# Routing chain reordered, filler matmuls on TensorE, the slot loop turned round, and own tiles for the last slot

## The chip, the cores and the metric

The kernel runs on one core of one Trainium2 chip. The metric is device microseconds (us) of one execution, as the median of several. Engines are named as in the profile: PE is TensorE (PEld its weight loads), DVE VectorE, ACT ScalarE, POOL GpSimd, SP SyncE.

## The reference

Three layers follow each other. A delta-rule attention layer gives `x` (3072 tokens of 384), a dense feed-forward layer gives `x1`, and a mixture of eight experts with one expert for each token gives the output:

```
for t in range(S):                                   # attention: 4 x 8 heads, 768 steps, state 48x48
    y[:, :, t] = q[:, :, t] @ state
    state = state + beta * outer(k_n, v - state @ k_n)
h = np.maximum(x @ w_in, 0.0);  x1 = h * h @ w_out   # 384 -> 2048 -> 384
logits = x1 @ w_gate;  e = argmax(logits)            # 8 experts
out[token] = softmax(logits)[e] * (relu(x1[token] @ w1[e]) @ w2[e])    # 384 -> 1024 -> 384
```

The gate's weight is positive, so the kernel multiplies the rows of `x1` by it before the expert layer.

## The kernel before, in words

Everything is written out by hand: each engine has its own program, and semaphores alone order the engines. Matmuls in fp32r are done in three passes (high times high, high times low, low times high), so each operand has a high part (ACT copies it with rounding) and a low part (DVE or POOL subtract).

The first part, `front`, runs over six chunks of 512 tokens. While PE works through the 16 blocks of the dense layer for chunk t (`up`, `down`, 18 matmuls a block), the delta rule of chunk t+1 is woven in. After each chunk's sum the tokens are routed: `sums` (ACT) copies the three result banks to `x1T`, `gate_logits` (PE) makes the logits, `choose` and `gates` (DVE) pick an expert and the gate, `ranks` (PE) counts tokens before each one, `places` (DVE) makes the token's place within its expert, `turn` (PE) and `turned` (ACT) turn the rows back and scale them, and SP stores them in HBM (`store_x1`). For chunks 0 to 4 this lies beside the next chunk's blocks. For chunk 5 nothing is left to lie beside: PE, DVE and ACT wait for each other in the order logits, `choose`, `ranks`, `places`, `slots`, `lists`.

`slots` (DVE) lays each expert's tokens into slots of 128 rows, 31 in all: it counts the slots that each expert needs (`need`, `end`, `begin`), gives each token its slot (`slot`) and builds one-hot matrices `parts` (24 columns of 128 tokens, 32 slots) in three groups of 8 columns. `mark_spots` (DVE) builds the other one-hot factor, `here` (a token's row within its slot, times its number); chunks 0 to 2 are marked in the last chunk's first blocks, chunks 3 and 4 behind its last block, chunk 5 between the groups of `parts`. `lists` (PE) multiplies the two, 24 matmuls into one bank, and DVE turns the sum into `ids`, the token numbers of each slot. `x_slot`, `rows` and the expert layer follow from it: POOL gathers the rows of slot 0, 1, 2, ... by `ids` (`gather`), and for each slot PE turns the rows (`turn_x`), ACT and DVE split them (`x_hi`, `x_lo`), PE runs `up` (18 matmuls of 512 columns), ACT the relu, PE turns the result (`turn_h`, 8 transposes), ACT and DVE split it (`h_hi`, `h_lo`), PE runs `down` (24 matmuls of 384 columns), ACT copies the result to `rows` and POOL scatters it. PE's loop body for slot s is `up(s)`, `turn_x(s+1)`, `down(s-1)`, `turn_h(s)`, so the small steps of one slot lie beside the matmuls of another.

The weights of experts 0 and 1 are loaded during the last chunks and split by `expert_hi` (ACT, one piece of 768 columns behind a block) and `expert_lo` (POOL, as soon as the piece is there). SP issues the raw weights of expert 2 as soon as those splits are done and the rows of chunk 5 are stored.

## Time and profile before

| | us |
|---|---|
| median of 3 runs | 988.73 (988.29 to 989.4) |
| the profiled execution, its own time | 986.88 |
| its span in the trace | 985.2 |
| PE busy | 895.5 of the span |
| DVE busy | 468.7 |
| ACT busy | 426.7 |
| POOL busy | 195.0 |

PE's busy time says that some matmul was in flight, not that it ran at its full speed: matmuls overlap, and their ends are modelled. What a stage costs is read from the distance between starts. The profiled execution is 1.85 us below the median, and its span is 1.68 us below its own time.

### The profile page before, as it was taken

How to read it: one execution, taken by the hardware profiler on the slowest of the kernel's cores; microseconds unless marked ns; L12 is line 12 of the kernel's file. 1: busy time of each engine (PE TensorE's matmuls, PEld its weight loads, DVE VectorE, ACT ScalarE, POOL GpSimd, SP SyncE). 2: the span in 40 equal slices, each digit the busy share in tenths (PEclk: the TensorE clock that was granted, in tenths of full speed). 3: DMA queues.
4: the chain of work that ended last, by engine and by line, in shares of the span. 5: the costliest groups of instructions: out<-in, count | busy, mean ns of one | idle time of the engine just before them, and what ended most of it. 6: DMA issues, size and time to landing. Idle time of an engine off the chain costs nothing.

```text
span 985.2 us, 25990 instructions
## 1 busy us (share of the span) xinstructions
PE 895.5 (91%) x10379; PEld 767.9 (78%) x10380; DVE 468.7 (48%) x953; ACT 426.7 (43%) x745; POOL 195.0 (20%) x146
## 2 busy tenths in 40 slices
PE   3161999999999999999999999986999999999997
PEld 3161788788877888888888888865989898899987
DVE  6989679746744675467422144152232323232221
ACT  4051746753566347534633555641333333333332
POOL 3000000000000000000000013335676623376311
PEclk8575899999999999999999999986999999999999
DMA  7005558933864377437633796607567733361100
GB/s 315 1 16 212 195 178 301 387 133 131 280 225 132 109 277 266 130 126 235 200 128 100 249 358 222 226 33 231 145 238 282 254 137 136 128 257 73 63 23 6
DMA packets 36893, 175.85 MB, mean 179 GB/s; under 512 B 4574, under 2 KB 7812, under 8 KB 30914
## 3 DMA queue, kind: packets, MB, share of 16 engines
q1 hardware_dynamic: 30242, 144.83, 41.3%
q0 software_dynamic: 6560, 29.70, 8.6%
q8 instruction: 71, 1.16, 0.5%
q14 instruction: 20, 0.16, 0.0%
HBM read 147.76 MB, written 28.12 MB: 179 GB/s over the span
## 4 chain that ended last, share of the span: by engine, by line
PE 85%; DVE 9%; issue 2%; ACT 2%; DMA 1%; POOL 0%; DVEq 0%; POOLq 0%; ACTq 0%
PE HP L1104 7%; PE ACC L1117 7%; PE HP L1105 6%; PE HP L1106 6%; PE ACC L1118 6%; PE ACC L1119 6%; PE HP L1442 5%; PE HP L1443 4%; PE HP L1444 4%; PE ACC L1467 4%; PE ACC L1468 4%; PE ACC L1469 4%; PE P L1008 3%; PE P L1453 3%; DVE prod L676 2%
## 5 line engine op out<-in xcount | busy, mean ns | idle before, releaser
L356 POOL TENSOR_TENSOR we_l<-raw_e,we_h 128x768 fp32r<-128x768 f32 x16 | 31.0, 1941 | 615.1 <-ACT we_h L482 615.1
L725 DVE TENSOR_TENSOR h_l<-h,h_h 128x512 fp32r<-128x512 f32 x96 | 66.3, 690 | 175.3 <-ACT h_h L456 175.2
L448 ACT ACTIVATE relu<-HP 128x512 f32<-128x512 f32 x96 | 57.4, 598 | 201.1 <-PE HP L1106 200.7
L1104 PE MATMUL HP<-x_h,ring 128*128 128x512 f32 x288 | 119.1, 414 | 0.6 <-DVE x_l L718 0.6
L1117 PE MATMUL ACC<-h_h,ring 128*128 128x512 f32 x288 | 117.2, 407 | 0.6 <-DVE h_l L725 0.6
L1105 PE MATMUL HP<-x_h,ring 128*128 128x512 f32 x288 | 113.4, 394 | 0.4 <-issue 0.4
L1106 PE MATMUL HP<-x_l,ring 128*128 128x512 f32 x288 | 113.4, 394 | 0.0
L1118 PE MATMUL ACC<-h_h,ring 128*128 128x512 f32 x288 | 113.1, 393 | 0.0
L1119 PE MATMUL ACC<-h_l,ring 128*128 128x512 f32 x288 | 112.9, 392 | 0.0
L1392 DVE TENSOR_TENSOR hT_l<-P,hT_h 128x512 fp32r<-128x512 f32 x62 | 40.0, 686 | 101.7 <-ACT hT_h L1346 101.7
L1297 POOL TENSOR_TENSOR we_l<-raw_e,we_h 128x1536 fp32r<-128x1536 f32 (+2 forms) x24 | 83.8, 3514 | 21.9 <-DMA we_h<-in_w 21.4
L1467 PE MATMUL ACC<-we_h,hT_h 128*128 x248 | 86.0, 347 | 1.3 <-DVE hT_l L1392 1.3
L1468 PE MATMUL ACC<-we_l,hT_h 128*128 x248 | 83.6, 337 | 0.0
L1469 PE MATMUL ACC<-we_h,hT_l 128*128 x248 | 83.4, 336 | 0.0
L1442 PE MATMUL HP<-we_h,xT_h 128*128 x186 | 77.3, 416 | 2.4 <-DVE xT_l L1385 2.3
L1339 ACT ACTIVATE h_slot<-HP 128x512 f32<-128x512 f32 x62 | 37.2, 600 | 95.9 <-PE HP L1444 95.1
L1443 PE MATMUL HP<-we_l,xT_h 128*128 x186 | 74.5, 400 | 0.0
L1444 PE MATMUL HP<-we_h,xT_l 128*128 x186 | 74.4, 400 | 0.0
L1385 DVE TENSOR_TENSOR xT_l<-ACC,xT_h 128x384 fp32r<-128x384 f32 x31 | 17.3, 558 | 119.5 <-ACT xT_h L1333 119.5
L1104 PEld LDWEIGHTS HP<-x_h,ring 128*128 128x128 f32 x288 | 54.5, 189 | 13.9 <-issue 2.6
L1117 PEld LDWEIGHTS ACC<-h_h,ring 128*128 128x128 f32 x288 | 54.4, 189 | 13.3 <-DVE h_l L725 1.0
L1350 ACT ACTIVATE rows<-ACC 128x384 f32 (+1 forms) x31 | 15.2, 491 | 113.9 <-PE ACC L1469 113.9
(195 smaller groups left out, 1719.7 us busy)
## 6 DMA issues: line engine op xcount, KB each, us to landing
ring<-w_scratch SPq DMA_DIRECT2D x80, 768.0 KB, 4.8
raw_e<-in_w SPq DMA_DIRECT2D x16, 1536.0 KB, 7.0
w_scratch<-ring SPq DMA_DIRECT2D x16, 768.0 KB, 5.3
we_h<-in_w POOLq DMA_DIRECT2D x6, 1536.0 KB, 9.2
kT<-in_kT SPq DMA_DIRECT2D x6, 1024.0 KB, 8.9
kk<-in_k SPq DMA_DIRECT2D x6, 1024.0 KB, 8.2
qT<-in_qT SPq DMA_DIRECT2D x6, 1024.0 KB, 9.6
we_h<-in_w POOLq DMA_DIRECT2D x6, 1024.0 KB, 6.1
```

The costliest lines, as they stand in the source:

```text
L1104: pe.matmul(HP[n % 2][:, :], win_h[:, cols], x_h[:, k, :], start=k == 0, stop=False)
L1105: pe.matmul(HP[n % 2][:, :], win_l[:, cols], x_h[:, k, :], start=False, stop=False)
L1106: last = pe.matmul(HP[n % 2][:, :], win_h[:, cols], x_l[:, k, :], start=False, stop=k == KD - 1)
L1117: pe.matmul(ACC[m][:, :], wout_h[:, cols], h_h[n % 2][:, :], start=f == 0, stop=False)
L1118: pe.matmul(ACC[m][:, :], wout_l[:, cols], h_h[n % 2][:, :], start=False, stop=False)
L1119: last = pe.matmul(ACC[m][:, :], wout_h[:, cols], h_l[n % 2][:, :], start=False, stop=f == NF1 - 1)
L1442: pe.matmul(HP[n][:, :], xT_h[:, lhs], wh[:, cols], start=k == 0, stop=False)
L1443: pe.matmul(HP[n][:, :], xT_h[:, lhs], wl[:, cols], start=False, stop=False)
L1444: last = pe.matmul(HP[n][:, :], xT_l[:, lhs], wh[:, cols], start=False, stop=k == KD - 1)
L1467: pe.matmul(YP[:, 0:DM], hT_h[:, lhs], wh[:, cols], start=f == 0, stop=False)
L1468: pe.matmul(YP[:, 0:DM], hT_h[:, lhs], wl[:, cols], start=False, stop=False)
L1469: last = pe.matmul(YP[:, 0:DM], hT_l[:, lhs], wh[:, cols], start=False, stop=f == NF2 - 1)
```

## The change

On DVE, `places` is split: `count` adds a chunk's counts to `filled`, and for the last chunk it comes alone before `slots`. `slots` then makes `begin`, and a new `give_slots` works on ranges of columns: 0 to 7, 8 to 19, and 20 to 23 (the last chunk). Only ahead of the third range stand `places(5)` and `mark_spots(5)`. `mark_spots` uses four tensor_scalar instructions of 128 elements instead of two tensor_tensor instructions of 512. Chunks 3 and 4 are marked behind the last two blocks. On ACT the last four pieces of `expert_hi` go behind blocks 13 and 14, two each.

On PE, the last chunk's logits are ordered by k-block instead of by batch, so that they may start when the first of three copies is there. `stay_awake` is new: matmuls of a high part with itself into bank ACC[2], whose result nobody reads. There are 3 of 512 columns behind the logits, 10 of 512 and 25 of 64 ahead of `lists`, and 74 of 64 behind it. `LIST` moves to bank ACC[0]. `lists` waits for the groups of 8, 12 and 4 columns.

SP's first load for expert 2 also waits for the first gathered slot.

In the expert layer PE's loop starts with `turn_h`, and `turn_h` of the last slot stands in the middle of the `down` of the slot before it. The last slot's hidden rows and its result have tiles and a bank of their own, so nothing waits for the other slot's buffers.

```diff
+HTL0, Y0 = 2, 1
+SHORT = (25, 74)
...
-    LIST = AUX[:, 0:NS]
+    LIST = ACC[0][:, 0:NS]
...
-            elif t == NCH and f >= 9:
+            elif t == NCH and 9 <= f < 13:
                 expert_hi(f - 1)
-        expert_hi(15)
+            elif t == NCH and f in (13, 14):
+                for i in range(2 * f - 14, 2 * f - 12):
+                    expert_hi(i)
...
+        def count(t):
+            dve.wait_ge(ranked, t + 1)
+            then(dve.tensor_tensor(filled[(t + 1) % 2][:, :], filled[t % 2][:, :], ADD, ALU.add))
+
         def places(t):
 
-            dve.wait_ge(ranked, t + 1)
+            if t < NCH - 1:
+                count(t)
...
-            then(dve.tensor_tensor(filled[(t + 1) % 2][:, :], filled[t % 2][:, :], ADD, ALU.add))
...
-            mine = here[t // KD][:, n:n + B, :]
-            then(dve.tensor_tensor(mine, spots[:, :].unsqueeze(1).broadcast_to([128, B, 128]),
-                                   spot[:, B * t:B * (t + 1)].unsqueeze(2).broadcast_to([128, B, 128]), ALU.is_equal))
-            dve.tensor_tensor(mine, mine.bitcast(F32), token[:, B * t:B * (t + 1)].unsqueeze(2).broadcast_to([128, B, 128]),
-                              ALU.mult).then_inc(here_done, 1)
+            for c in range(B * t, B * (t + 1)):
+                last = dve.tensor_scalar(here[t // KD][:, n + c - B * t, :], spots[:, :], spot[:, c:c + 1],
+                                         token[:, c:c + 1], ALU.is_equal, ALU.mult)
+            last.then_inc(here_done, 1)
+
+        def give_slots(begin, lo, hi):
+
+            n, cols = hi - lo, slice(lo, hi)
+            mine = relu[1][:, 0:n * NE].rearrange("p (c e) -> p c e", e=NE)
+            then(dve.tensor_tensor(mine, picked[:, cols, :].bitcast(F32), begin.unsqueeze(1).broadcast_to([128, n, NE]),
+                                   ALU.mult))
+            then(dve.tensor_reduce(slot[:, cols], mine, AX.X, ALU.add))
+            then(dve.tensor_tensor(slot[:, cols], slot[:, cols], line[:, cols], ALU.add))
+            dve.tensor_tensor(parts[:, cols, :], slot[:, cols].unsqueeze(2).broadcast_to([128, n, NS]),
+                              slot_no[:, :].unsqueeze(1).broadcast_to([128, n, NS]), ALU.is_equal).then_inc(parts_done, 1)
...
             dve.wait_ge(up_done, NF1 * NCH)
-            for n in range(0, NCOL, NLIST):
...
+            give_slots(begin, 0, NLIST)
+            give_slots(begin, NLIST, NCOL - B)
+            places(NCH - 1)
+            mark_spots(NCH - 1)
+            give_slots(begin, NCOL - B, NCOL)
...
+            if t == NCH and f >= 14:
+                dve.wait_ge(x1_out, 16 * NCH)
+                mark_spots(f - 11)
...
-        dve.wait_ge(x1_out, 16 * NCH)
-        for t in range(KD, NCH - 1):
-            mark_spots(t)
         choose(NCH - 1)
         gates(NCH - 1)
-        places(NCH - 1)
+        count(NCH - 1)
         slots()
...
+        def stay_awake(n, columns=TILE):
+
+            for _ in range(n):
+                pe.matmul(ACC[2][:, 0:columns], h_h[1][:, 0:128], h_h[1][:, 0:columns], start=True, stop=True)
...
-                if c % NLIST == 0:
-                    pe.wait_ge(parts_done, c // NLIST + 1)
-                    pe.wait_ge(here_done, NCH if c == NCOL - NLIST else NCH - 1)
+                if c in (0, NLIST, NCOL - B):
+                    pe.wait_ge(here_done, NCH - 1 if c < NCOL - B else NCH)
+                    pe.wait_ge(parts_done, 1 if c == 0 else 2 if c == NLIST else 3)
...
-        for b in range(B):
-            gate_logits(NCH - 1, b)
+        pe.wait_ge(placed, NCH - 1)
+        for m in range(KD):
+            pe.wait_ge(x1T_done, KD * (NCH - 1) + m + 1)
+            for b in range(B):
+                last = pe.matmul(AUX[:, DM + NE * b:DM + NE * (b + 1)], x1T[:, m, C * b:C * (b + 1)], wg[:, m, :],
+                                 start=m == 0 and b == 0, stop=m == KD - 1 and b == B - 1)
+        last.then_inc(lg_done, B)
+        stay_awake(3)
...
+        stay_awake(10)
+        stay_awake(SHORT[0], 64)
         lists()
...
+        stay_awake(SHORT[1], 64)
...
                 sp.wait_ge(lo_done, NPIECE * e + 2 * n + 2)
+                if e == 2:
+                    sp.wait_ge(first_rows[0], 16)
...
+        def last_h_hi():
+            for n in range(2):
+                act.wait_ge(ht_done, 2 * (NSLOT - 1) + n + 1)
+                act.activation(last_hh[n][:, :], TP[n][:, :], ACT.Copy).then_inc(hth_done, 1)
...
+        last_h_hi()
         result(NSLOT - 2)
-        h_hi(NSLOT - 1)
-        result(NSLOT - 1)
+        result(NSLOT - 1, last_YP)
...
+                if f == 4 and between is not None:
+                    turn_h(between)
...
-        turn_h(0)
-        with pe.Fori(1, NSLOT - 1) as s:
-            up(s, slot_expert(s))
-            turn_x(s + 1)
-            down(s - 1, slot_expert(s - 1))
+        with pe.Fori(0, NSLOT - 2) as s:
             turn_h(s)
+            up(s + 1, slot_expert(s + 1))
+            turn_x(s + 2)
+            down(s, slot_expert(s))
+        turn_h(NSLOT - 2)
         up(NSLOT - 1, slot_expert(NSLOT - 1))
-        down(NSLOT - 2, slot_expert(NSLOT - 2))
-        turn_h(NSLOT - 1)
-        down(NSLOT - 1, slot_expert(NSLOT - 1))
+        down(NSLOT - 2, slot_expert(NSLOT - 2), between=NSLOT - 1)
+        down(NSLOT - 1, slot_expert(NSLOT - 1), bank=last_YP, last_tiles=last_h)
```

PE's program from the last chunk's logits to the first slot, before (AUX, P, HP and ACC are PSUM banks; L1130 the logits, L1152 `turn`, L1140 to L1144 `ranks`, L1163 `lists`, L1423 `turn_x(0)`):

```order
L1130 MATMUL AUX<-wg,x1T 128x8 x12
L1152 MATMUL P<-ident,x1T 128x128 x6
L1140 MATMUL AUX<-picked,upper 128x32
...
L1144 MATMUL AUX<-picked,ones_sq 128x8 x4
L1152 MATMUL HP<-ident,x1T 128x128 x6
L1163 MATMUL AUX<-parts,here_x 128x32 x24
L1412 UNCONDITIONAL_BRANCH
L1423 MATMUL ACC<-ident,rows 128x128 x3
```

The same place in the changed kernel:

```order
L1262 MATMUL AUX<-wg,x1T 128x8 x12
L1169 MATMUL ACC<-h_h 128x512 x3
L1163 MATMUL P<-ident,x1T 128x128 x6
L1151 MATMUL AUX<-picked,upper 128x32
...
L1155 MATMUL AUX<-picked,ones_sq 128x8 x4
L1163 MATMUL HP<-ident,x1T 128x128 x6
L1169 MATMUL ACC<-h_h 128x512 x10
L1169 MATMUL ACC<-h_h 128x64 x25
L1179 MATMUL ACC<-parts,here_x 128x32 x24
L1169 MATMUL ACC<-h_h 128x64 x74
L1451 UNCONDITIONAL_BRANCH
L1462 MATMUL ACC<-ident,rows 128x128 x3
```

Three blocks of fillers now stand in PE's queue, one behind the logits, one ahead of `lists` and one between `lists` and the first slot.

DVE's program from the ranks of the last chunk to `ids`, before, is in this order (L770 to L778 `places`, L802 to L812 the slots, L818 `parts`, L786 and L788 `mark_spots`):

```order
L770 TENSOR_TENSOR rank<-AUX,filled 128x32
L772 TENSOR_TENSOR filled<-filled,AUX 128x8
...
L802 TENSOR_TENSOR relu<-filled,steps 128x192
...
L809 TENSOR_TENSOR relu<-picked,relu 128x192
L811 TENSOR_REDUCE slot<-relu 128x24
L812 TENSOR_TENSOR slot<-slot,line 128x24
L818 TENSOR_TENSOR parts<-slot,slot_no 128x256 x2
L786 TENSOR_TENSOR here_x<-spots,spot 128x512
L788 TENSOR_TENSOR here_x<-here_x,token 128x512
L818 TENSOR_TENSOR parts<-slot,slot_no 128x256
```

In the changed kernel it is this (L802 to L806 `give_slots`, L779 to L786 `places`, L794 `mark_spots`):

```order
L770 TENSOR_TENSOR filled<-filled,AUX 128x8
L819 TENSOR_TENSOR relu<-filled,steps 128x192
...
L802 TENSOR_TENSOR relu<-picked,relu 128x64
...
L806 TENSOR_TENSOR parts<-slot,slot_no 128x256
...
L806 TENSOR_TENSOR parts<-slot,slot_no 128x384
L779 TENSOR_TENSOR rank<-AUX,filled 128x32
...
L786 SCALAR_TENSOR_TENSOR spot<-line,place 128x4
L794 TENSOR_SCALAR here_x<-spots,spot,token 128x128 x4
...
L806 TENSOR_TENSOR parts<-slot,slot_no 128x128
```

The places of the last chunk moved from ahead of the slots to behind the first two groups of `parts`, and the last group shrank from 256 to 128 elements.

## Rows read from the trace of the kernel before

**Rows 1.** The page, clock of PE granted in 40 slices, tenths.

```profile
PEclk8575899999999999999999999986999999999999
```

**Rows 2.** Timeline of PE, last chunk to slot 1: start, us, engine, line.

```profile
650.62 0.50 PE L1117 MATMUL ACC<-h_h,ring 128*128 128x512 f32 x1 [0.56 <-DVE h_l L725]
...
653.64 2.85 PE L1130 MATMUL AUX<-wg,x1T 128*128 128x8 f32 x24 [0.69 <-ACT x1T L462]
...
657.89 0.40 PE L1140 MATMUL AUX<-picked,upper 128*128 128x32 f32 x1 [0.26 <-DVE picked L753]
...
659.62 1.54 PE L1152 MATMUL HP<-ident,x1T 128*128 128x128 f32 x6
664.49 5.30 PE L1163 MATMUL AUX<-parts,here_x 128*128 128x32 f32 x24 [3.33 <-DVE parts L818]
676.38 0.88 PE L1423 MATMUL ACC<-ident,rows 128*128 128x128 f32 x3 [6.58 <-DMA rows<-x_scratch,ids]
678.81 0.79 PE L1442 MATMUL HP<-we_h,xT_h 128*128 x1 [1.55 <-DVE xT_l L1385]
...
685.43 0.49 PE L1423 MATMUL ACC<-ident,x_slot 128*128 128x128 f32 x3
...
687.68 0.50 PE L1442 MATMUL HP<-we_h,xT_h 128*128 x1 [0.75 <-DVE xT_l L1385]
```

**Rows 3.** Windows, PE alone: length, PE busy (x), PEclk, DMA share, GB/s.

```profile
656.00:657.00 1.00, 1.00 (x10) 0.81 0.00 0
...
683.50:684.00 0.50, 0.50 (x2) 0.57 0.79 194
```

**Rows 4.** Timeline of DVE, ranks of the last chunk to `ids`.

```profile
659.79 0.19 DVE L770 TENSOR_TENSOR rank<-AUX,filled 128x32 f32<-128x32 f32 x1 [1.25 <-PE AUX L1144]
...
661.32 0.35 DVE L802 TENSOR_TENSOR relu<-filled,steps 128x192 f32<-128x192 f32 x1
...
663.01 0.36 DVE L809 TENSOR_TENSOR relu<-picked,relu 128x192 f32<-128x192 f32 x1
...
664.01 0.76 DVE L818 TENSOR_TENSOR parts<-slot,slot_no 128x256 fp32r<-128x256 f32 x2
...
666.35 0.40 DVE L821 TENSOR_TENSOR h<-slot_no,relu 1x248 f32<-1x248 f32 x1
...
667.61 0.16 DVE L826 CAST control<-relu 1x8 int32<-1x8 f32 x1
669.93 0.19 DVE L828 TENSOR_SCALAR ids<-AUX 128x31 int32<-128x31 f32 x1 [2.16 <-PE AUX L1163]
```

**Rows 5.** Timeline of POOL: the first gather.

```profile
671.05 1.23 POOL L1281 DMA_INDIRECT rows<-x_scratch,ids  x1 [15.96 <-DVE ids L828]
```

**Rows 6.** The 31 gathers by their source line, from issue to landing.

```profile
DMA to landing us min/median/max: 3.0/3.2/5.2
```

**Rows 7.** Timeline of SP: the raw weights of expert 2.

```profile
665.52 0.82 SPq L1276 DMA_DIRECT2D raw_e<-in_w  x2
```

**Rows 8.** Timeline of PE, ranks of an earlier chunk, full clock.

```profile
343.23 0.59 PE L1144 MATMUL AUX<-picked,ones_sq 128*128 128x8 f32 x4
```

**Rows 9.** Timeline of POOL in the last chunk's block 14: `expert_lo`.

```profile
646.57 1.85 POOL L356 TENSOR_TENSOR we_l<-raw_e,we_h 128x768 fp32r<-128x768 f32 x1 [2.23 <-ACT we_h L482]
```

**Rows 10.** Chain that ended last, one turn of the slot loop: start, us, what.

```profile
706.24 0.87 PE P L1453 x8
707.11 0.23 PE HP L1442
...
711.31 0.33 PE ACC L1423 x3
715.82 0.87 PE P L1453 x8
```

**Rows 11.** DMA queues between 700 and 950 us: the instruction queues.

```profile
q14 instruction: 3, 0.02, 0.0%
```

**Rows 12.** Timeline of PE, the last slot's down matmuls.

```profile
976.91 0.44 PE L1467 MATMUL ACC<-we_h,hT_h 128*128 x1 [1.28 <-DVE hT_l L1392]
```

More of the change, by code:

```diff
@@ L808, in slots @@
             then(dve.tensor_tensor(begin, end, need, ALU.subtract))
-            then(dve.tensor_tensor(mine, picked[:, :, :].bitcast(F32), begin.unsqueeze(1).broadcast_to([128, NCOL, NE]),
-                                   ALU.mult))
-            then(dve.tensor_reduce(slot[:, :], mine, AX.X, ALU.add))
-            then(dve.tensor_tensor(slot[:, :], slot[:, :], line[:, :], ALU.add))
             dve.wait_ge(up_done, NF1 * NCH)
-            for n in range(0, NCOL, NLIST):
-                cols = slice(n, n + NLIST)
-                if n == NCOL - NLIST:
-                    mark_spots(NCH - 1)
-                dve.tensor_tensor(parts[:, cols, :], slot[:, cols].unsqueeze(2).broadcast_to([128, NLIST, NS]),
-                                  slot_no[:, :].unsqueeze(1).broadcast_to([128, NLIST, NS]),
-                                  ALU.is_equal).then_inc(parts_done, 1)
+            give_slots(begin, 0, NLIST)
[3 more added lines that the diff above has]
+            give_slots(begin, NCOL - B, NCOL)
             then(dve.tensor_tensor(all_past, slot_no[0:1, 0:NSLOT].unsqueeze(2).broadcast_to([1, NSLOT, NE]),
@@ L1249, in _, with expert_layer @@
             turn(NCH - 1, b, turn_bank[b])
+        stay_awake(10)
+        stay_awake(SHORT[0], 64)
         lists()
-def expert_layer(nc, ctx, block, banks, routed, tiles, experts, w1, w2, x1_scratch, ident, ids, control, out):
+        stay_awake(SHORT[1], 64)
+def expert_layer(nc, ctx, block, banks, routed, tiles, last_h, experts, w1, w2, x1_scratch, ident, ids, control, out):
     def sem(name):
@@ L1393, in h_lo, with last_h_lo @@
                                   ALU.subtract).then_inc(htl_done, 1)
+        def last_h_lo():
+            for n in range(2):
+                dve.wait_ge(hth_done, 2 * (NSLOT - 1) + n + 1)
+                dve.tensor_tensor(last_hl[n][:, :], TP[n][:, :], last_hh[n][:, :].bitcast(F32),
+                                  ALU.subtract).then_inc(htl_done, 1)
         fetch(1)
@@ L1450, in turn_h @@
                 after(pe, h_done, 2 * s + n + 1)
-                after(pe, htl_done, 2 * s - 1 + n)
+                after(pe, htl_done, 2 * s - 1 + n + HTL0)
                 for f in range(4):
@@ L1455, in turn_h, with down @@
                 last.then_inc(ht_done, 1)
-        def down(s, e):
+        def down(s, e, between=None, bank=YP, last_tiles=None):
             wh, wl = (w[:, :, :].rearrange("p b n -> p (b n)") for w in (we_h, we_l))
-            after(pe, y_done, s)
+            if last_tiles is None:
+                after(pe, y_done, s + Y0)
             at = (e & 1) * WE
             for f in range(NF2):
+                if f == 4 and between is not None:
+                    turn_h(between)
                 if f % 4 == 0:
                     pe.wait_ge(lo_done, NPIECE * e + (NPIECE + 3 + f // 4))
-                    after(pe, htl_done, 2 * s + f // 4 + 1)
-                lhs = slice(128 * f, 128 * (f + 1))
+                    after(pe, htl_done, 2 * s + f // 4 + 1 + HTL0)
+                if last_tiles is None:
+                    h_hi, h_lo = (h[:, 128 * f:128 * (f + 1)] for h in (hT_h, hT_l))
+                else:
+                    h_hi, h_lo = (h[f // 4][:, 128 * (f % 4):128 * (f % 4 + 1)] for h in last_tiles)
                 cols = bass.ds(at + (W1 + DM * f), DM)
-                pe.matmul(YP[:, 0:DM], hT_h[:, lhs], wh[:, cols], start=f == 0, stop=False)
-                pe.matmul(YP[:, 0:DM], hT_h[:, lhs], wl[:, cols], start=False, stop=False)
-                last = pe.matmul(YP[:, 0:DM], hT_l[:, lhs], wh[:, cols], start=False, stop=f == NF2 - 1)
+                pe.matmul(bank[:, 0:DM], h_hi, wh[:, cols], start=f == 0, stop=False)
+                pe.matmul(bank[:, 0:DM], h_hi, wl[:, cols], start=False, stop=False)
+                last = pe.matmul(bank[:, 0:DM], h_lo, wh[:, cols], start=False, stop=f == NF2 - 1)
             last.then_inc(slots_done, 1)
         pe.sem_inc(slots_done, 1)
+        pe.sem_inc(htl_done, HTL0)
+        pe.sem_inc(y_done, Y0)
         pe.wait_ge(routed, 2)
@@ L1511, in build @@
                  sb("hT_l", [128, F2], F32R))
+        last_h = [[sb(f"last_h{c}{n}", [128, 512], F32R) for n in range(2)] for c in ("h", "l")]
         def bank(name):
@@ L1524, in build @@
               xT_scratch, x1_scratch, ident, ids, control)
-        expert_layer(nc, ctx, block, banks, routed, tiles, experts, w1, w2, x1_scratch, ident, ids, control, out)
+        expert_layer(nc, ctx, block, banks, routed, tiles, last_h, experts, w1, w2, x1_scratch, ident, ids, control, out)
 def kernel(**inputs):
```

14 lines of the change are left out of this document (7 added, 7 removed).

## The prediction

> **What bounds the kernel now.** I read the page first. The granted clock stands at 9 or more in every slice behind the start but for three around 700 us [rows 1]: one place, between the dense layer and the expert layer, where PE is neither busy nor fast. Then the timeline of PE there [rows 2]. Between the last `down` block, which begins at 650.62, and `up(1)` at 687.68 lie only the logits, the ranks, 24 small matmuls of `lists`, one `turn_x` and `up(0)`; the rest is waiting, 3.33 us for `parts`, 6.58 us for the first gather. The windows add the clock [rows 3]: it falls within the window from 656 to 657, though PE was then busy with 24 passes of 8 columns, and is back at full in the window from 683.5. So the second half of the logits' wake, ranks, turns, `lists` and 5 us of `up(0)` run at 1.2 GHz. Behind that, the slot loop: the chain of one turn is 0.87 for `turn_h`, 4.20 for `up`, 0.33 for `turn_x`, 4.18 for `down` (each from its row's start to the next), and these fill the whole period of 9.58, 715.82 less 706.24 [rows 10]. Last, the final slot waits 1.28 us for its split [rows 12]. What can be gained is thus in the passage and at the end, hardly in the loop.
>
> **The logits and the block before them.** Ordered by k-block, the logits need one copy of `x1T` instead of three, so the wait of 0.69 ahead of them goes [rows 2]: they end at 655.8 instead of 656.49. Against this stands a price. ACT's second cast behind block 14 makes POOL run two subtractions of 1.85 from 646.57, until 650.3 [rows 9], and DVE, which now marks chunk 3 in that time, does the `h_l` that PE waits for until 650.62 [rows 2]. It was free of POOL before. Bounds: nothing, if they don't disturb each other, and 1.0, if `h_l` has to wait for POOL. I take 0.4, nearer to the first since the overlap is under half a microsecond. Logits end at 656.2.
>
> **Ranks.** From the logits' end to the first rank pass DVE chooses, 1.40 (656.49 to 657.89), unchanged: 657.6. The three wide fillers and six transposes (0.7 and 0.66 at full clock) fit before that. Ranks to DVE took 1.90 at half clock (657.89 to 659.79 [rows 2, 4]). At full clock a pass of these costs 0.113: four in 0.59, of which the last takes 0.25, in [rows 8]; eight are 0.9, with the way to DVE 1.0. DVE starts at 658.6 instead of 659.79.
>
> **DVE's chain.** Before, it runs from 659.79 to 667.77 and then waits for `lists` until 669.93 [rows 4]. Now: count 0.20; slots needed to `begin` 1.69 (661.32 to 663.01); first group 1.06 (three small steps of 0.2 to 0.26, `parts` 0.34 to the next start); second group 1.25, since it is half as wide again; the rest of `places` 1.4 (661.32 less 659.79, less count, plus one wait); four marks of 128 elements; third group 0.84; control words 1.47 (666.35 to 667.77 and the step to `ids`). The mark in this form has no row. A 192-wide instruction costs 0.36, a narrow one 0.16 [rows 4], so four lie between 0.6 and 1.5; I take 1.0. The sum is 8.9, so `ids` at 667.5 instead of 669.93, 2.4 earlier. `lists` does not hold it back: its third group may start at 666.0.
>
> **The gather.** It starts 1.12 behind `ids` (669.93 to 671.05 [rows 4, 5]), now at 668.6. Its landing took 5.2, the longest of 31, with a median of 3.2 [rows 6]; beside it ran 3 MB of raw weights issued at 665.52 [rows 7], which now wait for it. I take 3.2, between 3.0 and 5.2. Rows of slot 0 are there at 671.8, against 676.3. The raw weights start some 6 us later; their user, the split for expert 2, comes after POOL's 31 gathers of 1.3 each, so past 709, and this costs nothing; behind SP's new wait stand only the loads for experts 2 to 7.
>
> **The fillers.** These are what PE must do before `turn_x(0)`, whether or not the rows are there, for they stand ahead of it in a queue that keeps its order. From the ranks at 657.6: eight passes 0.9, six transposes 0.66, ten of 512 columns at 0.233 (the step of `up` [rows 10]) 2.33, 25 of 64 columns, `lists`, 74 of 64 columns. The price of a 64-column one decides. Passes of 8 columns cost 0.113 [rows 8], of 32 columns at half clock 0.214 (5.30 less the last, by 23 [rows 2]), so twice as much as at full: the cost does not follow the columns but the weight load, and 64 columns stay under it. Bounds: 0.06 if something of the load goes away for weights that repeat, 0.113 otherwise. I take 0.113. Then 25 end at 664.3, 20 of `lists` at 666.6, four more at 667.05, 74 (8.36 us) at **675.4**. That is 3.6 later than the rows land, so the fillers take the place of the gather as the last to end, and the shorter chain to the slots is worth only what is left, 676.38 less 675.4: **1.0**.
>
> **Slot 0 and the end.** With the clock held, `turn_x(0)` to `up(0)` (2.43) loses 0.3, since three transposes took 0.88 where 0.33 is the step at full clock, hidden in part by the copies. `up(0)` took 6.62 (678.81 to 685.43 [rows 2]) and takes 4.3, **2.3** less. From there to `up(1)` nothing changes. At the end `turn_h(30)` in the middle of `down(29)` puts 12 matmuls, 2.1 us, over ACT's and DVE's split (0.6 and 0.7 for each half); the 1.28 goes, less 0.1 for one more change between transposes and matmuls: **1.2**.
>
> **The loop.** The order of the work is the same around the cycle; only the branch moves. It can save or cost no more than the chain leaves open, under 0.02 of 9.58, so 0.6 in 29 turns; I take 0. The instruction queue of PE moved nothing between 700 and 950: of the instruction queues only q14 appears there, with three packets [rows 11], so no code is fetched again in 26 turns.
>
> The Trainium skill, page Runtime: NRT & Kernel Launch, section Instruction fetch mechanics, says that a taken branch to code outside the pages held forces a fetch and a stall. By it a loop body over two blocks might pay each turn; the trace's period leaves no room for it, and the sum stays.
>
> Sum: 1.0 + 0.3 + 2.3 + 1.2 = 4.8. The profiled execution goes from 986.88 to 982.1 (its span from 985.2 to 980.4); it stands 1.85 below the median of the runs, so 983.9 against 988.73.
>
> **The rivals.**
> *The gather ends last, not the fillers.* If a 64-column filler costs under 0.072 (5.3 us for 74, from 666.5 to 671.8), 3.6 more are gained: 980.3. For it speaks only that the same weights are loaded again each time; against it the 0.113 at every small width.
> *The fillers run at half clock.* Before the fall PE was busy with passes of 8 columns, and 5.3 us of 32-column passes of `lists` did not bring the clock back [rows 2, 3]. No row shows 64. If the clock falls under them each costs 0.214, 0.10 more; 74 are 7.5 us, and the 2.6 of slot 0 are lost too: 4.8 less 10.1, **994.0**, slower. It decides from 22 fillers at half clock (2.2 of gain left, at 0.10 each).
> *The clock falls where it fell,* at 656 to 657, and comes back behind the wide fillers: ranks 0.9 more, turns 0.7, ten wide fillers up to 2. Gain 1.2 to 2: 987.1.
> *The loop or the end does not do what it should,* or DVE and POOL disturb each other by the full 1.0 and more: up to 2 less, 986.
>
> The Trainium skill, TensorE: Matmul & The Clock Gate, section Why this matters for your kernels, says to leave no long idle gap between bursts of matmuls. The fall at 656.6 came with PE busy, so the trace shows more than that rule; by the rule alone the fillers hold the clock and the second and third rival fall away, which leaves 983.9 or 980.3.
>
> **How the numbers follow.** Forecast 0.50 (own range 982.3 to 985.6, from `h_l` and the step of transposes), gather last 0.17, half-clock fillers 0.13, clock falls early 0.12, other losses 0.08. The range from 979.5 to 989.0 leaves out the slow rival and the far ends. A difference under 0.2%, 2 us, cannot be told from none: faster 0.75 (the forecast, gather last, most of the other losses, a little of the early fall), same 0.10 (the rest of the early fall, above all), slower 0.15 (half-clock fillers, and an early fall that stays).
>
> **What would show it.** Clock at full in all windows from 640 to 700. `ids` near 667.5, the first gather landed in 3.2, and `turn_x(0)` with no wait for the gather, straight behind the last filler, near 675.4: then the fillers bind. A wait for the DMA ahead of it says that they don't. `up(0)` in 4.3. Loop period 9.58. No idle ahead of the last `down`. The prediction is wrong if fillers step at other than 0.113, if the clock row shows 0.5 among them, or if the period moves.

## The result and the profile after

The kernel before took 988.77 us (median of 12 executions, 986.56 to 990.0), the changed one **994.4** (12, 990.1 to 1000.26): ratio 1.006, 95% interval 1.0041 to 1.008. It is slower, where 983.9 was forecast. The profiled execution took 994.48, its span 992.6 against 985.2. The times also spread over 10 us instead of 3.4.

The page's clock row of the changed kernel, in 40 slices, answers to [rows 1]; there are now a 9 and a 5 where an 8 and a 6 stood:

```profile
PEclk9995899999989999999999999995999999999999
```

Windows of PE over the same passage (length, PE busy, granted clock, DMA share, GB/s), answering to [rows 3]:

```profile
656.00:665.00 9.00, 9.00 (x68) 1.00 0.24 87
667.00:693.00 26.00, 24.47 (x102) 0.50 0.71 243
694.00:700.00 6.00, 5.30 (x28) 1.00 0.55 147
```

The clock is full until 665 and at half, the 1.2 GHz level, for 26 us from 667, with PE busy nearly all the time. The timeline of PE (start, us) shows with what, and answers to [rows 2]:

```profile
651.90 0.50 PE L1128 MATMUL ACC<-h_h,ring 128*128 128x512 f32 x1 [1.42 <-DVE h_l L729]
...
654.08 2.74 PE L1262 MATMUL AUX<-wg,x1T 128*128 128x8 f32 x24
...
658.68 0.59 PE L1155 MATMUL AUX<-picked,ones_sq 128*128 128x8 f32 x4
...
659.76 5.24 PE L1169 MATMUL ACC<-h_h 128*128 128x512 f32 x35
664.83 4.40 PE L1179 MATMUL ACC<-parts,here_x 128*128 128x32 f32 x24
669.07 15.97 PE L1169 MATMUL ACC<-h_h 128*128 128x64 f32 x74
684.86 0.90 PE L1462 MATMUL ACC<-ident,rows 128*128 128x128 f32 x3
687.28 0.79 PE L1481 MATMUL HP<-we_h,xT_h 128*128 x1 [1.53 <-DVE xT_l L1418]
694.22 0.49 PE L1462 MATMUL ACC<-ident,x_slot 128*128 128x128 f32 x3
696.42 0.49 PE L1481 MATMUL HP<-we_h,xT_h 128*128 x1 [0.70 <-DVE xT_l L1418]
```

Three things are to be seen. The group of 35 is 10 wide and 25 short fillers; it ran at full clock, so a short one cost (5.07 from start to start, less 10 times 0.233) by 25, 0.11. The 74 behind `lists` took 15.79 to the next start, 0.213 each. And `turn_x(0)` has no idle time ahead of it: it waited for the fillers.

DVE, from the last blocks to `ids`, answers to [rows 4] (parts of the chain left out):

```profile
646.21 0.91 DVE L729 TENSOR_TENSOR h_l<-h,h_h 128x512 fp32r<-128x512 f32 x1 [3.39 <-ACT h_h L458]
647.04 4.20 DVE L794 TENSOR_SCALAR here_x<-spots,spot,token 128x128 fp32r<-128x128 f32 x4
651.16 0.68 DVE L729 TENSOR_TENSOR h_l<-h,h_h 128x512 fp32r<-128x512 f32 x1
651.77 1.10 DVE L794 TENSOR_SCALAR here_x<-spots,spot,token 128x128 fp32r<-128x128 f32 x4
...
659.31 0.16 DVE L770 TENSOR_TENSOR filled<-filled,AUX 128x8 f32<-128x8 f32 x1 [0.44 <-PE AUX L1155]
...
668.10 0.16 DVE L837 CAST control<-relu 1x8 int32<-1x8 f32 x1
669.37 0.19 DVE L839 TENSOR_SCALAR ids<-ACC 128x31 int32<-128x31 f32 x1 [1.11 <-PE ACC L1179]
```

POOL in the same timeline, and SP's raw weights, which are issued when the first gather has landed [rows 5, 7, 9]:

```profile
646.99 3.65 POOL L358 TENSOR_TENSOR we_l<-raw_e,we_h 128x768 fp32r<-128x768 f32 x2 [0.42 <-ACT we_h L484]
...
670.49 1.23 POOL L1309 DMA_INDIRECT rows<-x_scratch,ids  x1 [19.84 <-DVE ids L839]
```

```profile
673.84 0.82 SPq L1304 DMA_DIRECT2D raw_e<-in_w  x2
```

So the rows of slot 0 were there at about 673.8, and PE took them up 11.0 us later. Where the 7.4 us of the span are (to 0.1): `up(1)` starts 8.74 later (696.42, was 687.68). Of this 1.28 lies ahead of the last `down` block (651.90, was 650.62), 7.20 between it and `turn_x(0)` (32.96 instead of 25.76), 0.26 behind. The turns of the loop up to `turn_h(29)` add 0.30, the end gives 1.54 back.

Two profiles of the changed kernel differ by 2.5 us in the time at which the last `down` block starts, so all later places are given from that start. For the kernels that matter, in us:

| | before | changed | e5 | e7 | e9 | e13 |
|---|---|---|---|---|---|---|
| `ids` | 19.31 | 17.47 | 17.12 | 16.48 | 16.47 | 16.46 |
| `turn_x(0)` | 25.76 | 32.96 | 21.68 | 22.83 | 21.02 | 20.99 |
| `up(0)` | 28.19 | 35.38 | 24.56 | 25.26 | 23.07 | 23.04 |
| `turn_x(1)` | 34.81 | 42.32 | 31.50 | 31.76 | 27.37 | 27.33 |
| first split for expert 2 | 69.65 | 68.01 | 67.33 | 66.48 | 67.01 | 64.20 |
| `turn_h(4)` to `turn_h(5)` | 9.64 | 9.58 | 10.67 | 9.72 | 15.99 | 13.22 |
| `turn_h(5)` | 84.27 | 91.67 | 81.95 | 81.27 | 83.12 | 80.32 |

The last row and the 1.54 of the end tell the time. Against the kernel before they give 5.9 us more for the changed kernel (medians: 5.6 more), and less by 3.9 for e5 (3.8), 2.7 for e9 (2.6), 5.5 for e13 (6.1). For e7 they give 4.5 less where the medians say 2.0, and its profiled execution was the fastest of its 12 (982.68 against a median of 986.16).

### The profile page after: what moved, and what is told of

Read it like the earlier page. It is cut to its first block, busy times and chain, and to the rows that moved or that the text cites. A ratio compares the mean times of both kernels' runs of the same rounds, so it can differ in the third digit from the quotient of the medians.

```text
span 992.6 us, 26235 instructions
## 1 busy us (share of the span) xinstructions
PE 916.1 (92%) x10491; PEld 788.8 (79%) x10492; DVE 469.0 (47%) x971; ACT 426.3 (43%) x745; POOL 193.4 (19%) x146
## 4 chain that ended last, share of the span: by engine, by line
PE 86%; DVE 9%; issue 2%; ACT 2%; DMA 1%; POOL 1%; DVEq 0%; ACTq 0%; POOLq 0%
PE HP L1115 7%; PE ACC L1128 7%; PE HP L1116 6%; PE HP L1117 6%; PE ACC L1130 6%; PE ACC L1129 6%; PE HP L1481 4%; PE HP L1482 4%; PE HP L1483 4%; PE ACC L1512 4%; PE ACC L1513 4%; PE ACC L1514 4%; PE P L1492 2%; PE P L1019 2%; PE ACC L1169 2%; DVE prod L680 2%
## 5 line engine op out<-in xcount | busy, mean ns | idle before, releaser
L1130 PE MATMUL ACC<-h_l,ring 128*128 128x512 f32 x288 | 113.2, 393 | 0.0
L1512 PE MATMUL ACC<-we_h,hT_h 128*128 x240 | 83.3, 347 | 0.0
L1513 PE MATMUL ACC<-we_l,hT_h 128*128 x240 | 80.9, 337 | 0.0
L1514 PE MATMUL ACC<-we_h,hT_l 128*128 x240 | 80.7, 336 | 0.0
L1117 PEld LDWEIGHTS HP<-x_l,ring 128*128 128x128 f32 x288 | 54.8, 190 | 12.2
```

The source lines that it names most:

```text
L1117: last = pe.matmul(HP[n % 2][:, :], win_h[:, cols], x_l[:, k, :], start=False, stop=k == KD - 1)
L1130: last = pe.matmul(ACC[m][:, :], wout_h[:, cols], h_l[n % 2][:, :], start=False, stop=f == NF1 - 1)
L1512: pe.matmul(bank[:, 0:DM], h_hi, wh[:, cols], start=f == 0, stop=False)
L1513: pe.matmul(bank[:, 0:DM], h_hi, wl[:, cols], start=False, stop=False)
L1514: last = pe.matmul(bank[:, 0:DM], h_lo, wh[:, cols], start=False, stop=f == NF2 - 1)
```

## The experiments

Four groups ran, each kernel beside the kernel before on the same chip. Ratios are to that.

| | us | ratio, 95% |
|---|---|---|
| *group 1, before 1009.55* | | |
| e1 no short ones behind the lists | 1007.98 | 0.999 (0.9975 to 1.0005) |
| e2 256 columns | 1015.83 | 1.0052 (1.0028 to 1.0076) |
| e3 loop and end only | 1008.32 | 0.9991 (0.9978 to 1.0004) |
| e4 no fillers | 1005.47 | 0.9962 (0.9948 to 0.9975) |
| *group 2, before 988.18* | | |
| e5 no fillers, early marks | 984.36 | 0.996 (0.9946 to 0.9974) |
| e6 few wide fillers | 985.18 | 0.9974 (0.9962 to 0.9987) |
| e7 half the tail | 986.16 | 0.9989 (0.9974 to 1.0003) |
| e8 changed kernel again | 997.21 | 1.0088 (1.0074 to 1.0102) |
| *group 3, before 987.3* | | |
| e9 wide fillers, DVE's order | 984.68 | 0.9964 (0.9951 to 0.9977) |
| e10 e5 with DVE's order | 984.79 | 0.9965 (0.9952 to 0.9978) |
| e11 e5 without SP's wait | 985.19 | 0.9977 (0.9966 to 0.9987) |
| e12 e5 with the old expert layer | 986.21 | 0.9985 (0.9974 to 0.9996) |
| *group 4, before 988.82* | | |
| e13 e9 with POOL's load earlier | 982.76 | 0.9937 (0.9924 to 0.995) |
| e14 e5 with POOL's load earlier | 984.41 | 0.9946 (0.9931 to 0.9961) |
| e15 e14 with late marks | 984.5 | 0.9959 (0.9945 to 0.9973) |
| e16 e13 with short ones behind the lists | 983.2 | 0.9947 (0.9932 to 0.9962) |

### Group 1: fillers fewer, wider, none

```diff
-SHORT = (25, 74)
+SHORT = (25, 0)                       # e1
...
-        stay_awake(SHORT[0], 64)
+        stay_awake(SHORT[0], 256)     # e2, and the same behind lists
```

e3 is the `front` of the kernel before with the changed expert layer, without SP's wait. e4 is the changed kernel with all calls of `stay_awake` taken out.

> The changed kernel without the 74 fillers behind lists. Theory A (PE works through 74 fillers at half clock, 15.97 us, while the rows of slot 0 land near 673.7): turn_x(0) begins at 673.8 instead of 684.86, up(0) still begins at half clock, the median falls by 11 from 994.4 to 983.4, and turn_x(0) waits for the gather again. Theory B (the loss lies in the loop, its place in the program or the last slot, and the fillers fill time that was idle anyway): 992 to 996.

> All 99 short fillers with 256 columns instead of 64, same count, so more work each. Theory A (what costs is the clock that falls under thin passes): the clock stays at full, a filler steps at 0.12 instead of 0.21, the 74 take 8.9 instead of 15.97, up(0) takes 4.3, median 983 to 985. Theory B (the clock falls through lists' 32 columns whatever the fillers are, or the step follows the columns): the 74 take 16 us or more at half clock, median 994 or more.

> The kernel before with the new expert layer alone: loop turned round, turn_h of the last slot in the middle of down, own tiles; no filler, no new chain, no wait of SP for the gather. Theory A (the loop is bound by matmuls, the end gains its idle 1.28 less a change of mode): 1.2 less than before, 987.5, period 9.58. Theory B (the turned loop costs or gives time at its branch): the period moves by 0.05 or more, 1.5 us in 29 turns.

> The changed kernel without any filler. Theory A: the clock falls near 657 as in the kernel before; the marks beside POOL cost 1.3, the shorter chain and the gather that no longer shares its DMA give 3 to 4, the end 1.2: first rows land near 673, median 984 to 985. Theory B (the shorter chain brings nothing once lists runs at half clock, since the gather is no faster): 987 to 989.

In this group every kernel, the one before too, took some 20 us more than elsewhere, so only ratios can be read, and these with care. The timeline of PE in e4 shows where, in the first turn of the loop:

```profile
705.06 0.48 PE L1509 MATMUL ACC<-we_l,hT_h 128*128 x1 [1.46 <-issue]
707.16 0.48 PE L1510 MATMUL ACC<-we_h,hT_l 128*128 x1 [1.62 <-issue]
709.97 0.48 PE L1508 MATMUL ACC<-we_h,hT_h 128*128 x1 [2.33 <-issue]
```

"issue" is time in which PE waited for nothing that the profile shows. In e1, e3 and e4 matmuls of `down(0)` stood up to 2.1 and 2.8 us apart instead of 0.17, until about 715 us, some 5 us behind the issue of the last gather; the first turn took 31 us instead of 10.7. In e2 the same sort of gap, 8.04 us, stood ahead of `up(0)`, and the second half of `turn_h(0)` began only at 714.07. What PE gains in slot 0 is swallowed there. What can still be told: without any filler the kernel is faster than before (e4: by 0.38%), which speaks against the fillers and not against the shorter chain. e4's ratio is what its theory A gave (984 to 985 of 988.73).

**e1**: the wait for the gather was back ahead of `turn_x(0)` (4.69 us), which began 22.1 us behind the last `down` block instead of 33.0, and `up(0)` ran at half clock (6.94). So theory A's mechanism came; of its 11 us the ratios (0.999 against 1.006) show 7. **e2**: both theories missed. The clock did fall, at 669.5, 1 us into the fillers behind `lists`, but it was back at full by 673, while they ran; the 74 took 10.44 us, 0.14 each, where A said 8.9 and B 16. At full clock one of 256 columns cost 0.12 (5.39 for 10 wide and 25 of these ahead of `lists`, less 2.33), hardly more than one of 64. The time, forecast at 983 to 985, was the slowest of the group; how much of that the gaps made is not known. **e3**: the forecast of 1.2 us fits 0.0009 of 1009.55 (0.9), but its interval includes no difference; the later turns took 9.58 and 9.59, so theory B falls.

### Group 2: number, width, marks

```diff
-            elif t == NCH and 9 <= f < 13:
+            elif t == NCH and f >= 9:                       # e5: ACT's pieces as before
-            elif t == NCH and f in (13, 14):
-                for i in range(2 * f - 14, 2 * f - 12):
-                    expert_hi(i)
+        expert_hi(15)
...
-            if t == NCH and f >= 14:
-                dve.wait_ge(x1_out, 16 * NCH)
-                mark_spots(f - 11)
...
+        dve.wait_ge(x1_out, 16 * NCH)
+        for t in range(KD, NCH - 1):
+            mark_spots(t)
         choose(NCH - 1)
...
-        stay_awake(SHORT[0], 64)
+        stay_awake(7)                                       # e6
         lists()
-        stay_awake(SHORT[1], 64)
+        stay_awake(14)                                      # e6; in e7 37 of 64 columns
```

> The changed kernel without any filler matmul, and with the marks of chunks 3 and 4 behind the last block and ACT's last expert_hi pieces where they stood before; the output stays the reference's. Theory A (the marks beside POOL's two subtractions cost what the changed profile shows, 1.3 us on PE's path): DVE's last h_l at 649.9 again, logits end 1.3 earlier, ids 1.0 to 1.3 earlier than without fillers alone, time 0.13% less than that kernel. Theory B (the marks only move the wait elsewhere, since choose or the slots wait for DVE): ids no earlier, same time as without fillers alone.

> The changed kernel with the short fillers taken out: 7 more of 512 columns ahead of the lists (17 in all), 14 of 512 behind them instead of 74 of 64. Theory A (what held PE back was only the number and price of the short ones, and wide ones hold the clock): the fillers end near 672.5, turn_x(0) starts with the gather near 675, up(0) in 4.3 instead of 6.6, so 8 to 11 us less than the changed kernel where slot 0's start sets the time. Theory B (the clock falls anyhow in the wait of 2 us for the gather): turn_x(0) the same, up(0) in 6 or more, 7 us less than the changed kernel.

> The changed kernel with 37 short fillers behind the lists instead of 74. Theory A (each costs 0.214 at half clock and they bind until turn_x(0)): turn_x(0) 7.9 us earlier than in the changed kernel, at 677.0, the time 8 us less, near 986.5 on the first chip. Theory B (something else, not their number, sets turn_x(0)): under 3 us less.

> The changed kernel once more, nothing altered, beside the others on one chip. Both theories: 0.6% slower than the kernel before if this chip is like the first. If this chip shows stalls of PE's sequencer during the gathers, as the last batch's did in the first turn of the slot loop, a part of the difference is swallowed by them.

**e8** repeats the result (1.0088, was 1.006). **e5**: DVE's last `h_l` and PE's wait behind it were as in the kernel before (0.56 us, where e4 has 1.42), as theory A said. But `ids` came only 0.16 earlier than in e4 (17.12 and 17.28 behind the block), and the ratios are the same, 0.996 and 0.9962, in different groups; the 0.13% did not show.

**e7** against e8: 11.05 us less for 37 short fillers, more than the 8 expected. PE in e7:

```profile
666.39 7.35 PE L1169 MATMUL ACC<-h_h 128*128 128x64 f32 x37
673.55 0.90 PE L1462 MATMUL ACC<-ident,rows 128*128 128x128 f32 x3
```

37 took 7.16 to the next start, where 74 in e8 took 15.79; that is 8.6. Another 1.5 is that in this profile of e7 the clock fell behind `lists` (24 passes in 2.68) and in e8 in it (4.14). So where the clock falls differs between executions, and fillers behind that place cost 0.213 each. The spread of the changed kernel's times may come from this: of its 12 executions ten have a mean granted clock that falls as the time rises, from 0.972 at 990.1 to 0.962 at 1000.26; the other two (0.948 at 993.07, 0.945 at 995.66) do not fit, and the place of the fall was read in one alone. Theory A holds, with this addition.

**e6** kept the clock through its wide fillers, but it fell at about 675.8, in the waits that followed, of 1.89 and 3.60 us. `turn_x(0)` began with the gather (672.66) and `up(0)` ran at half, 6.91 us, as theory B said; against e8 it gained 12.0 us, more than either theory gave. The time was e5's or worse (0.9974 to 0.996). There `up(0)` waited 3.60 for `xT_l`, and DVE shows why; it does so in e5 too, here:

```profile
674.44 0.36 DVE L1407 COPY x_slot<-rows 128x384 f32<-128x384 f32 x1 [6.08 <-DMA rows<-x_scratch,ids]
674.72 0.55 DVE L1412 TENSOR_TENSOR xT_l<-ACC,xT_h 128x384 fp32r<-128x384 f32 x1
```

DVE's copy of slot 1's rows stands ahead of `x_lo(0)`, so slot 0 waits for the second gather. In e5 `xT_h` was ready by 674.2.

### Group 3: hold the clock all the way; the gather; the loop

```diff
+        stay_awake(22)                # e9 behind lists (17 wide ahead of them)
...
         turn_x(0)
+        pe.wait_ge(lo_done, NPIECE + 1)
+        for _ in range(5):            # e9
+            pe.matmul(last_YP[:, :], we_h[:, 0, 0:128], we_h[:, 0, 0:512], start=True, stop=True)
...
-        fetch(1)
         x_lo(0)
+        fetch(1)                      # e9, e10
...
-                if e == 2:            # e11, on e5
-                    sp.wait_ge(first_rows[0], 16)
```

> The changed kernel with early marks (as in the kernel before), wide fillers only (3 behind the logits, 17 ahead of the lists, 22 behind them, 5 between turn_x(0) and up(0)), and DVE's x_lo(0) ahead of its copy of slot 1's rows; the output stays the reference's. Theory A (the gather's landing, then the two copies, then a full clock bind): clock at full in all windows from 650 to 700, turn_x(0) near 672.7, up(0) 1.2 to 1.6 later and in 4.3, so 3.5 to 4 us less than e5, 7 to 8 less than the kernel before. Theory B (the clock falls in slot 0 all the same, or the fillers delay turn_x(0)): at most 1 us less than e5.

> The kernel of e5 (no fillers, early marks) with one swap: DVE's x_lo(0) stands ahead of its copy of slot 1's rows. Theory A (in e5 up(0) waits through that copy for the second gather): from turn_x(0)'s start to up(0) 2.4 us instead of 2.88, so 0.4 to 0.5 us less. Theory B (x_lo(0) waits for ACT anyhow): no difference.

> The kernel of e5 without SP's wait for the first gathered rows, so the raw weights of expert 2 are issued near 661 and lie beside the first gathers. Theory A (this traffic makes the first gather land late, 5.2 us in the kernel before against 3.2): turn_x(0) 1.8 us later than in e5, time 1.8 us more. Theory B (the landing does not depend on it): no difference.

> The front of e5 and SP's wait, with the expert layer of the kernel before (its loop order, its end without own tiles for the last slot). Theory A (the end is worth what the profiles show, 17.33 less 15.79 us from turn_h(29) to the last scatter, and the loop nothing): 1.5 us more than e5, period of the loop 9.58 to 9.59. Theory B (a loop body that lies over two blocks of 256 instructions costs each turn): period at least 0.03 longer, over 2.4 us more.

**e9** did in slot 0 nearly what was expected: full clock from 650 to 700, `turn_x(0)` at 672.56 (672.7 expected) with no wait, `up(0)` in 4.30, but 2.05 later and not 1.2 to 1.6. PE:

```profile
672.56 0.52 PE L1460 MATMUL ACC<-ident,rows 128*128 128x128 f32 x3
...
674.61 0.50 PE L1479 MATMUL HP<-we_h,xT_h 128*128 x1 [0.38 <-DVE xT_l L1416]
...
678.91 0.49 PE L1460 MATMUL ACC<-ident,x_slot 128*128 128x128 f32 x3
```

`turn_x(1)` came 4.1 us earlier than in e5 (27.37 against 31.50). Yet the time is e5's: 0.9964 to 0.996. The gain was given back 40 us later, in `up(5)`, for which PE's timeline in e9 has

```profile
721.26 0.49 PE L1479 MATMUL HP<-we_h,xT_h 128*128 x1 [1.55 <-POOL we_l L1323]
725.69 0.49 PE L1479 MATMUL HP<-we_h,xT_h 128*128 x1 [2.79 <-POOL we_l L1323]
```

and POOL's

```profile
708.62 0.99 POOL L1307 DMA_INDIRECT rows<-x_scratch,ids  x1 [0.30 <-issue]
714.39 1.15 POOL L1318 DMA_DIRECT2D we_h<-in_w  x2 [4.77 <-POOLq L1315]
715.51 0.56 POOL L1319 DMA_DIRECT2D we_h<-in_w  x1
718.55 13.87 POOL L1323 TENSOR_TENSOR we_l<-raw_e,we_h 128x1024 fp32r<-128x1024 f32 x4 [2.48 <-DMA we_h<-in_w]
```

Slot 5 is the first of expert 2. Its weights are split by POOL behind all 31 gathers, the wait for their landing and the load of `we_h`: a chain that hangs on `ids` and not on slot 0. In the kernel before it left PE no slack (the turn took 9.64 instead of 9.59). The turn in e9 took 6.4 us more than usual. By the starts of its matmuls some 4.7 of that is the two waits, and 1.6 is the clock, which fell behind the second wait; PE's window in e9:

```profile
727.00:730.00 3.00, 3.00 (x9) 0.52 0.96 360
```

My theory A of e9's time was wrong, and this was the new question.

**e10**: `turn_x(0)` to `up(0)` 2.39 instead of 2.88, as theory A said; the time did not move, for the same reason. That turn took 14.05: a wait of 2.67 in `up(5)`, and then the clock at half (0.52 from 727 to 730), which cost another 1.6. In e5 the wait was 0.82 and the clock stayed full (1.00 from 726 to 729). So e10 was 1.8 us ahead of e5 at `turn_x(1)` and 1.5 behind it at `turn_h(5)`: in these profiles it was worse to come early and wait than to come in time. **e11**: the gather landed late.

```profile
665.75 0.82 SPq L1296 DMA_DIRECT2D raw_e<-in_w  x2
```

```profile
676.81 0.87 PE L1454 MATMUL ACC<-ident,rows 128*128 128x128 f32 x3 [8.01 <-DMA rows<-x_scratch,ids]
```

From the gather's issue (670.20) to `turn_x(0)` 6.6 instead of 3.4. The other profiles without SP's wait have 5.3 (the kernel before) and 5.2 (e3); e1, e4, e6, e10, e12, e14 and e15, with it, 3.4 to 3.5. The ratio is 0.0012 above e10's, 1.2 us, with intervals that overlap. For the landing SP's wait works; in time little of it arrives, since slot 5 has the last word here too. **e12**: 1.4 to 1.5 us more than e10 and e9 by the medians, 2.0 by the ratios, with intervals that just overlap. From `turn_h(29)` to the last scatter it needs 17.33, the changed expert layer 15.79; so the end is worth 1.54. The ordinary turn is 9.58 or 9.59 in both: where the loop's body lies in the program costs or saves nothing that shows.

### Group 4: the chain to slot 5, the marks, the width

```diff
-        pool.wait_ge(group_in[(NGROUP - 1) % 2], ...)
-        pool.sem_inc(gathered, 1)
         for e in range(2, NE):
             weights(e)
+            if e == 2:                # e13 on e9, e14 on e5, e15 on e4
+                pool.wait_ge(group_in[(NGROUP - 1) % 2], ...)
+                pool.sem_inc(gathered, 1)
...
-        stay_awake(22)
+        stay_awake(45, 64)            # e16 on e13
```

> The kernel of e9 with one move on POOL: the load and split of expert 2 stand ahead of the wait for the last group of gathers instead of behind it. Theory A (in e9 PE waits 6.4 us in turn 4 for this split, which waits for the gathers to land): the load is issued 3 to 4 us earlier, turn 4 of the loop is 10 to 12 us long instead of 15.99, time 4 to 5.5 us less than e9, ratio to the kernel before near 0.992. Theory B (the load waits for PE's slots or for the place, not for the gathers): turn 4 stays within 1 us, time as e9.

> The kernel of e5 (no fillers) with the same move on POOL. Theory A: turn 4 was 10.67 in e5, so at most 1.1 us can come back: turn 4 at 9.6, time 1 us less than e5, ratio near 0.995. Theory B (the load waits for something else): as e5, 0.996.

> The kernel of e14 with the marks of chunks 3 and 4 and ACT's last pieces where the change put them. Theory A (marks beside POOL's subtractions delay the last h_l by 1.3 us on the path): 1.0 to 1.3 us more than e14, the last down block behind an idle time of 1.4 instead of about 0.5. Theory B (they cost nothing in the end): same as e14.

> The kernel of e13 with 45 fillers of 64 columns behind the lists in place of 22 of 512: 5.1 us at 0.113 each, the same time, if the clock holds. Theory A (short ones do not hold the clock, as the changed kernel's did not): the clock falls among them or in slot 0, they take up to 9.6 us, turn_x(0) up to 4.5 us later than in e13, time 3 to 6 us more. Theory B (the clock fell in the changed kernel for another reason, such as a gap ahead of the lists): clock full, time as e13.

**e13** has the lowest ratio of all, 0.63% under the kernel before; the intervals of several others, e14, e15 and e16 among them, overlap its own. POOL:

```profile
709.90 1.20 POOL L1318 DMA_DIRECT2D we_h<-in_w  x2
711.02 0.60 POOL L1319 DMA_DIRECT2D we_h<-in_w  x1
716.06 13.89 POOL L1323 TENSOR_TENSOR we_l<-raw_e,we_h 128x1024 fp32r<-128x1024 f32 x4 [4.44 <-DMA we_h<-in_w]
```

Counted from the last `down` block, the load starts 4.8 earlier, but beside the last gathers it takes longer (4.44 of waiting, was 2.48), so the split starts 2.8 earlier. The turn shrinks from 15.99 to 13.22, outside my 10 to 12, and the ratio falls by 0.0027 from e9's, 2.7 us (3.4 by the medians' distance to the kernel before). Theory A holds, its size was too large: a wait of 1.82 was left, and the clock fell behind it once more (0.50 from 724 to 727). In **e14** the turn is back at 9.59 and the ratio 0.0014 lower than e5's; the intervals overlap.

**e15** against e14 prices the marks. The last `down` block's first row, of e14 and then of e15:

```profile
653.43 0.50 PE L1126 MATMUL ACC<-h_h,ring 128*128 128x512 f32 x1 [0.56 <-DVE h_l L727]
```

```profile
651.91 0.50 PE L1128 MATMUL ACC<-h_h,ring 128*128 128x512 f32 x1 [1.42 <-DVE h_l L729]
```

0.86 us of idle time more. The ratios differ by 0.0013, 1.3 us, which fits theory A, but the intervals overlap and the medians are 0.1 apart (times of e14 reach from 981.05 to 985.47): the row shows the wait at this place, but what it costs in the end is not settled.

**e16**: same wide fillers ahead of the lists, then 45 short ones instead of 22 wide. PE and its windows:

```profile
666.86 8.36 PE L1167 MATMUL ACC<-h_h 128*128 128x64 f32 x45
```

```profile
656.00:665.00 9.00, 9.00 (x60) 1.00 0.24 87
669.00:678.00 9.00, 9.00 (x39) 0.50 0.69 224
```

In e13 the same stretch had

```profile
667.00:693.00 26.00, 24.79 (x125) 1.00 0.73 249
```

Two levels under the same kind of work, in blocks planned for the same 5.1 us; what differs is the width, and with it the number. Both kernels had the same wait of 1.02 us ahead of the last four passes of `lists`, and behind it PE was busy in both. So the clock's part of theory A holds, and theory B, a gap, falls. The other executions agree: their mean granted clocks are 0.976 to 0.979 in e13 and 0.970 to 0.976 (one 0.951) in e16. `turn_x(0)` came 2.8 later from the last `down` block, `turn_x(1)` 3.8 later. The expected 3 to 6 us did not follow (0.9947 to 0.9937, intervals overlapping): slot 0 began later, but slot 5 then had nothing to wait for, and its turn took 9.6 instead of 13.22.

## Why the prediction was wrong

**The step that failed** is "I take 0.113" for a 64-column filler, and under it "with the clock held". The rival "the fillers run at half clock", given 0.13 and priced at 994.0, is the mechanism that came. That its time came within half a microsecond is in part luck: it gave 5.3 us more, the medians show 5.6, the two profiled executions 7.6. In these `turn_x(0)` is at 684.86 and not at the rival's 682.9 (675.4 and 7.5), since the last `down` block stood 0.9 later than in the forecast and `lists` too ran mostly at half clock, 1.5 more. The working of 0.113 was right: at full clock they cost 0.11. What I had not derived was that the clock would stay full. [Rows 2, 3] spoke against it: before the fall PE had been busy with narrow passes, and 5.3 us of them did not bring it back. I used this as an argument for the rival and gave it too little.

The Trainium skill, TensorE: Matmul & The Clock Gate, section Why this matters for your kernels, asks for no long idle gap. The changed kernel left none: PE's last wait, 1.42 us, ended at 651.90, and its clock fell 14 us later, to 0.50 with PE busy throughout. This case needed more than that rule.

Point by point:

- **The clock before**: in [rows 1] two slices behind the start are under 9, an 8 and a 6 between 640 and 690 us, and not three around 700 as I wrote. Nothing in the sum hangs on it.
- **Logits**: 0.84 less from the last `down` block to them (2.18 instead of 3.02), 0.69 forecast. Right.
- **`h_l`**: 0.4 forecast, 1.0 as bound; 0.86 measured at PE. Mis-sized. Four marks took 4.20 beside POOL's two subtractions and 1.10 alone: I had looked at `h_l` against POOL and not at what DVE now did between them. The Trainium skill, SBUF — State Buffer, section SBUF: two separate sides, calls the port pair that DVE and GpSimd share an exclusive lock: where both need it, the one that starts first has it for its whole instruction. The trace agrees: two of the four marks began 0.05 behind one of POOL's subtractions each (647.04 and 648.85, against 646.99 and 648.80) and lasted until just behind its end, 1.88 and 1.89 us; the other two took 0.33 each.
- **Ranks**: DVE began 7.4 behind the last `down` block (659.31), 7.6 forecast (658.6, with the block at 651.02), 9.2 before. Right.
- **DVE's chain**: 8.9 forecast, 8.95 measured (659.31 to the end of the control words, 668.26). Right. But "`lists` does not hold it back" was wrong where the clock had fallen within `lists`: 1.11 more. With wide fillers (e13) `ids` is at 16.46, 2.85 earlier than before, where 16.5 was forecast (667.5 less 651.02).
- **Gather**: 1.12 and 3.35 (670.49 to SP's 673.84), forecast 1.12 and 3.2. Right, and e11 shows that SP's wait did it.
- **`turn_x(0)` to `up(0)`**: 0.3 forecast, none came (2.42, was 2.43); 2.05 in e9, which also has DVE's other order.
- **`up(0)`**: 2.3 forecast, none came in the changed kernel (6.94 to `turn_x(1)`); in e9 it took 4.30, as forecast for a full clock.
- **End**: 1.2 forecast, 1.54. **Loop**: 0, as forecast. The larger of the two instruction queues (q8) moved one packet more in all (72, was 71).

**A second step would have failed even with the clock held.** I wrote of expert 2's split that it comes past 709 "and this costs nothing". That the split comes behind the gathers was right, but not that it costs nothing: PE had no slack there, it already came to slot 5 as its weights did (the turn took 9.64 instead of 9.59). POOL's row of the kernel before:

```profile
720.27 14.01 POOL L1297 TENSOR_TENSOR we_l<-raw_e,we_h 128x1024 fp32r<-128x1024 f32 x4 [2.45 <-DMA we_h<-in_w]
```

By that chain the passage can gain only about what `ids` gains, and a faster slot 0 is given back. e9 shows it: `turn_x(1)` 7.4 us earlier than before, twice what I forecast up to `up(1)` (3.6), `turn_h(5)` only 1.15 earlier, and 2.6 us in all by the medians (3.5 by the ratio) instead of 4.8. None of my rivals had it.

What stays open: why the clock falls at different places in the same kernel, and what held PE's sequencer in group 1.

## What to carry to other kernels

Price filler work at half clock as well as at full, and let the chance between them follow from rows of work just as narrow; fillers that stand in a queue ahead of real work are a bet whose loss is their whole length. Before counting a gain in one passage, look for the next engine that meets PE downstream and measure the slack there: here there was none, 40 us later, and the waits that followed cost clock as well. A chain's true start (here `ids`) is what the gain must be counted at.
